# Two batches of local attention, a gated feed-forward stage and an ELU feed-forward stage: the second batch's attention issued among the first batch's feed-forward work

## The reference

```python
k_sum = k.reshape(B, H, 24, 32, D).max(axis=3)      # one key per block of 32
v_sum = v.reshape(B, H, 24, 32, D).mean(axis=3)
scores_l = scale * q @ k.T, kept where |i - j| < 16, else -1e9
scores_s = scale * q @ k_sum.T + log(32)
a = softmax(concat(scores_l, scores_s))             # over 768 + 24 keys
x = a @ concat(v, v_sum)                            # -> 1536 tokens x 512
h = x @ w_in                                        # 512 -> 1024
solu = h * softmax(h)
y = layernorm(solu) * g_ln @ w_out                  # 1024 -> 512
g = elu(y @ w2_in)                                  # 512 -> 2048
out = g @ w2_out                                    # 2048 -> 512
```

## Time and profile before

| | us |
|---|---|
| median of three runs | 532.42 |
| the three runs | 534.9, 532.42, 530.37 |
| profiled execution, its own time | 533.14 |
| its span in the trace | 531.4 |
| PE busy in the span | 495.5 |
| DVE, ACT, POOL busy | 234.9, 212.6, 100.5 |

### The profile page before, as it was taken

The page is one execution under the profiler, slowest core; times in us unless marked ns, Lnnn a source line. Parts: engine busy times, 40 slices in busy tenths (PEclk is TensorE's granted clock), DMA queues, the critical chain, the costliest instruction groups (busy, mean ns, idle before and its releaser), DMA issues.

```text
span 531.4 us, 8550 instructions
## 1 busy us (share of the span) xinstructions
PE 495.5 (93%) x3312; PEld 415.4 (78%) x3312; DVE 234.9 (44%) x625; ACT 212.6 (40%) x433; POOL 100.5 (19%) x92
## 2 busy tenths in 40 slices
PE   3769869896999999999999999999999999999997
PEld 2556757675879899899988888888888888888885
DVE  2536645634683454644265555433332323333331
ACT  2446746733573344544374435223222214122222
POOL 2245353510012002003444544100000000000000
PEclk9989977999999999999999999999999999999999
DMA  9999999661000000035000000002000002000002
GB/s 174 174 186 200 211 172 208 152 239 80 0 1 1 1 0 1 1 119 200 0 1 0 1 0 2 0 1 79 1 0 1 0 0 79 0 0 0 0 0 79
DMA packets 56131, 31.41 MB, mean 59 GB/s; under 512 B 50081, under 2 KB 50081, under 8 KB 55201
## 3 DMA queue, kind: packets, MB, share of 16 engines
q1 hardware_dynamic: 56096, 30.94, 25.5%
HBM read 26.61 MB, written 3.15 MB: 56 GB/s over the span
## 4 chain that ended last, share of the span: by engine, by line
PE 79%; SPq 8%; DMA 4%; DVE 3%; ACT 2%; issue 2%; POOL 1%; DVEq 0%
PE bank L825 12%; PE bank L826 12%; PE bank L827 12%; PE bank L1027 8%; PE bank L1026 8%; PE bank L1028 8%; PE bank L982 4%; PE bank L984 4%; PE bank L983 4%; DMA vw<-vmean 2%; PE bank L902 2%; SPq L275 2%; PE bank L968 2%; DMA vblocks<-in_v 2%; SPq L288 2%
## 5 line engine op out<-in xcount | busy, mean ns | idle before, releaser
L586 ACT ACTIVATE ex<-bank 128x512 f32<-128x512 f32 x48 | 28.7, 598 | 127.9 <-PE bank L827 127.9
L827 PE MATMUL bank<-yt_lo,w2in_hi 128*128 (+1 forms) x192 | 74.7, 389 | 0.0
L826 PE MATMUL bank<-yt_hi,w2in_lo 128*128 (+1 forms) x192 | 74.7, 389 | 0.0
L1026 PE MATMUL bank<-w2out_hi,g_hi 128*128 128x512 f32 x192 | 74.7, 389 | 0.0
L1027 PE MATMUL bank<-w2out_lo,g_hi 128*128 128x512 f32 x192 | 74.7, 389 | 0.0
L825 PE MATMUL bank<-yt_hi,w2in_hi 128*128 (+1 forms) x192 | 74.7, 389 | 0.0
L1028 PE MATMUL bank<-w2out_hi,g_lo 128*128 128x512 f32 x192 | 74.7, 389 | 0.0
L803 DVE TENSOR_SCALAR ex<-ex 128x512 f32<-128x512 f32 x48 | 21.6, 450 | 116.4 <-ACT ex L586 116.4
L808 DVE TENSOR_TENSOR g_lo<-gf,g_hi 128x512 fp32r<-128x512 f32 x48 | 46.5, 969 | 35.9 <-ACT g_hi L594 35.9
L594 ACT ACTIVATE g_hi<-gf 128x512 fp32r<-128x512 f32 x48 | 30.3, 632 | 49.0 <-DVE gf L805 49.0
L469 ACT ACTIVATE se<-se,nm 128x120 f32<-128x120 f32 x96 | 32.5, 387 | 38.6 <-DVE nm L654 38.6
(11 more groups left out here) (102 smaller groups left out, 820.3 us busy)
## 6 DMA issues: line engine op xcount, KB each, us to landing
w2in_raw<-in_w_in SPq DMA_DIRECT2D x1, 4096.0 KB, 12.4
w2out_raw<-in_w_out SPq DMA_DIRECT2D x4, 1024.0 KB, 9.4
kraw<-in_k SPq DMA_DIRECT2D x16, 192.0 KB, 4.1
qraw<-in_q SPq DMA_DIRECT2D x16, 192.0 KB, 4.1
vblocks<-in_v SPq DMA_DIRECT2D x4, 768.0 KB, 7.9
vw<-in_v SPq DMA_DIRECT2D x16, 192.0 KB, 5.6
out<-osb SPq DMA_DIRECT2D x12, 256.0 KB, 2.1
win_raw<-in_w_in SPq DMA_DIRECT2D x4, 512.0 KB, 6.1
```

The costliest lines, as they stand in the source:

```text
L826: pe.matmul(acc, al, bh, start=False, stop=False)
L827: last = pe.matmul(acc, ah, bl, start=False, stop=(i == n - 1))
L1026: pe.matmul(dst, g_hi[:, j % GS, cols], w2out_hi[:, j, :], start=(j == 0), stop=False)
```

## The change

The steps of attention stay, but from step 25 on they carry other work. Tables say at which step a row product (`ROWS_AT`), a pair of turns (`TURNS_AT`), a slice of y (`Y_AT`) and a group's factors (`STATS_AT`) are issued: rows 0 to 7, turns 0 to 15 and six of the eight y slices of groups 0 and 1 go into steps 25 to 50. Rows 8 to 11, the last two slices and turns 16 to 31 come after, in the manner of before. `y_slice(g, o)` is new: it makes one output slice of a group over all eight `f` in one go, 24 matmuls of 384 columns, in place of `y_product` after every turn.

For this, memory is laid out anew. From unit 25 on all scores go to one set of banks; the transposes of k, q and x are halved or kept at 384 columns, called pieces, and share a bank `psR`, which from step 36 on is the bank of `psP`; `psH`, `psT` and `psY` of groups 0 and 1 are one buffer each; `eh` has one buffer in place of two, `se` three in place of four, raw k and q together three in place of four, v two (a third for one pair). POOL normalises all rows; the order of the weights' DMAs is another.

```diff
+        def psS(u, h):
+            return bank(4 + h) if u < U0 and u % 2 == 1 else bank(h)
+        psO, psP = bank(2), bank(3)
+        def psR(u):
+            return bank(6 + u % 2) if u < U0 + T else bank(7) if u < U0 + 2 * T else bank(3)
+        def psH(m):
+            return banks[0] if m in (7, 9) else banks[2]
+        def psT(c):
+            return bank(2) if c >= 2 * KF and c % 2 == 1 else bank(6)
+        def psY(g, o):
+            return bank(7) if g < 2 else bank((7, 3, 0, 1)[o])
...
+        ROWS_AT = {25: 0, 27: 1, 29: 2, 31: 3, 33: 4, 37: 5, 49: 6, 50: 7}
+        TURNS_AT = {33: (0, 1), 34: (2, 3), 35: (4, 5), 36: (6, 7), 42: (8, 9), 43: (10, 11), 44: (12, 13), 45: (14, 15)}
+        Y_AT = {38: (0, 0), 39: (0, 1), 40: (0, 2), 41: (0, 3), 46: (1, 0), 48: (1, 1)}
+        SOLU_AT = {u + 1: m for u, m in ROWS_AT.items()}
+        STATS_AT = {31: 0, 39: 1}
+        AFTER = [(8, [(1, 2)], []), (9, [(1, 3)], [16]), (10, [], [17, 18]), (11, [], list(range(19, TURNS)))]
```

SP's loads of weights, in its loop over the pairs:

```diff
+                if n in (1, 2):
+                    load_win(2 * n - 2)
+                    load_win(2 * n - 1)
+                if n in (2, 3):
+                    load_vblocks(n)
+                if n in (3, 4):
+                    load_wout(2 * n - 6)
+                    load_wout(2 * n - 5)
```

ACT's step `u`; where it asks for a piece, `copy_k`, `copy_q` or `copy_x` of 384 columns follows:

```diff
+                if turns:
+                    high_turned(turns[0])
                 if u < UNITS:
                     exps(u)
                 if u >= T_LAG and u - T_LAG < UNITS and not pt_on_dve(u - T_LAG):
                     copy_pt(u - T_LAG)
+                if u in SOLU_AT:
+                    h_square(SOLU_AT[u])
+                if u in STATS_AT:
+                    deviation(STATS_AT[u])
+                if piece(u):
...
+                if turns:
+                    high_turned(turns[1])
+                if u in ROWS_AT:
+                    h_exp(ROWS_AT[u])
+                if u in Y_AT:
+                    high_y(*Y_AT[u])
```

DVE's step `u` has, each where the tables ask for it: `low_turned` of the first turn, `score(u)`, `row_solu`, `copy_pt(u-2)`, `normalise`, `variance`, `block_maxima`, `low_x`, `layernorm_factors`, `low_turned` of the second turn, `row_max`, `low_y`. PE's waits and its step (where it asks for a piece, `prep_k`, `prep_q` or `turn_x` into `psR(u)` follows):

```diff
             def scores(u):
...
                 if u >= 2:
-                    pe.wait_ge(scored, u - 1)
+                    pe.wait_ge(scored, u - 1 if u <= U0 else u)
...
             def turn_probs(u):
+                s, v = u % RING, u + T_LAG - 1
                 pe.wait_ge(expd, u + 1)
                 if u >= 1:
                     pe.wait_ge(*pt_copied(u - 1))
+                if v >= U0 + 2 * T and piece(v):
+                    pe.wait_ge(*piece_done(v))
...
             def turn(c):
...
+                if 1 <= c <= 2 * KF:
+                    pe.wait_ge(lnt_lo_ready, c)
...
+            def y_slice(g, o):
+                if g == 0 and o == 0:
+                    pe.wait_ge(wout_split, KF // 2)
+                else:
+                    pe.wait_ge(y_lo_ready, KD * g + o)
+                pe.wait_ge(lnt_lo_ready, KF * (g + 1))
...
+            for u in range(U_STEPS):
+                turns = TURNS_AT.get(u, ())
+                if turns:
+                    turn(turns[0])
+                if u < UNITS:
+                    scores(u)
+                if u >= T_LAG and u - T_LAG < UNITS:
+                    turn_probs(u - T_LAG)
+                if u >= PV_LAG and u - PV_LAG < UNITS:
+                    attend(u - PV_LAG)
+                if piece(u):
+                    kind, n, f = piece(u)
+                    if piece_before(u) is not None:
+                        pe.wait_ge(*piece_done(piece_before(u)))
+                    if u >= U0 + 2 * T:
+                        pe.wait_ge(*pt_copied(min(u - T_LAG, UNITS - 1)))
...
+                if u in ROWS_AT:
+                    rows_product(ROWS_AT[u], 0)
+                if turns:
+                    turn(turns[1])
+                if u in ROWS_AT:
+                    rows_product(ROWS_AT[u], 1)
+                if u in Y_AT:
+                    y_slice(*Y_AT[u])
```

More of the change, by code:

```diff
@@ L142, in bank @@
             return banks[i // 2][:, (i % 2) * 512:(i % 2) * 512 + 512]
[L144 to L156, removed]
+        def psS(u, h):
[9 more added lines that the diff above has]
+            return bank(7) if g < 2 else bank((7, 3, 0, 1)[o])
+        psG = [bank(4), bank(5)]
+        psA = [bank(6), bank(2), bank(7), bank(3)]
         def sem(name):
@@ L319, in _ @@
             load_k(1)
+            load_vblocks(1)
             load_q(1)
@@ L571, in _ @@
                     high_turned(c)
+                    if ends_group(c):
+                        for o in range(KD):
+                            high_y(c // KF - 1, o)
                     if TURNS - 6 <= c < TURNS - 1:
@@ L774, in _, with low_y @@
-            for m, turns in ROWS_AND_TURNS:
-                t = list(turns)
-                if m != TG + 1:
-                    row_max(m)
-                if m == TG:
-                    variance(0)
-                if t and not ends_group(t[0]):
+            def low_y(g, o):
+                tiles = slice(TG * g, TG * (g + 1))
+                dve.wait_ge(y_hi_ready, KD * g + o + 1)
+                dve.tensor_tensor(yt_lo[:, tiles, o, :], psY(g, o)[:, 0:GT].rearrange("p (t c) -> p t c", t=TG),
+                                  yt_hi[:, tiles, o, :].bitcast(F32), ALU.subtract).then_inc(y_lo_ready, 1)
@@ new lines, in _ @@
+            block_maxima(0)
+            dve.wait_ge(consts_ready, 2)
+            dve.wait_ge(vblocks_loaded[0], 16)
+            step(dve.tensor_reduce(vmean[:, 0, :], vblocks[:, 0, :].rearrange("p (w d) -> p d w", d=D), AX.X, ALU.add))
+            dve.tensor_scalar(vmean[:, 0, :], vmean[:, 0, :], 1.0 / BLOCK, None, ALU.mult).then_inc(first_vmean_ready, 1)
+            for u in range(U_STEPS):
+                n, t = u // T, u % T
+                turns = TURNS_AT.get(u, ())
+                if turns:
+                    low_turned(turns[0])
+                if u < UNITS:
+                    score(u)
+                if u in SOLU_AT:
+                    row_solu(SOLU_AT[u])
+                if u >= T_LAG and u - T_LAG < UNITS and pt_on_dve(u - T_LAG):
+                    copy_pt(u - T_LAG)
+                if u >= PV_LAG and (u - PV_LAG) % TG == TG - 1 and u - PV_LAG < UNITS:
+                    normalise((u - PV_LAG) // TG)
+                if u in STATS_AT:
+                    variance(STATS_AT[u])
+                if t == 3 and n + 1 < PAIRS:
+                    block_maxima(n + 1)
+                if u <= U0 and piece(u - 1) and piece(u - 1)[0] == "x":
+                    low_x(piece(u - 1)[1], psR(u - 1))
+                if u >= U0 and piece(u) and piece(u)[0] == "x":
+                    low_x(piece(u)[1], psR(u))
+                if u in STATS_AT:
+                    layernorm_factors(STATS_AT[u])
+                if turns:
+                    low_turned(turns[1])
+                if u in ROWS_AT:
+                    row_max(ROWS_AT[u])
+                if u in Y_AT:
+                    low_y(*Y_AT[u])
```

538 lines of the change are left out of this document (256 added, 282 removed).

## The result

The changed kernel took 589.36 us (median of four runs, 587.94 to 592.82) against 531.45: a ratio of 1.1105, 95% interval [1.1058, 1.1153]. The forecast was 556, range 538 to 570: the direction was right, the size too small by 33 us.

The account below looks back on a forecast made before the run. Attention was taken as bound by a PE, DVE, ACT, PE chain in list order, not PE's busy share. Batch 0 61, steps 24 to 51 159, after 70, second stage 264.7, outside 1.7: 556 us, range 538 to 570.

Parts of the forecast that it names:

- Reading past the busy share: Whole kernel: PE's 93% busy misleads; attention runs at a PE, DVE, ACT, PE chain, priced by the engines' lists.
- the first rival: Interleaved steps: waits vanish and PE stays the bound, 114 us there, 511 us in all; chance 0.13.
- Steps 24 to 51: Interleaved attention steps up to row 8: 159 us, of which 114 is PE's own work and the rest waiting.
- the clock: New waits in the interleaved steps: a lower clock would cost 0 to 5 us, taken as 0.
- The rest and the second stage: After step 51: 70 us to the second feed-forward stage, then 264.7 us for that stage, as before.
- 61 us, same units, smaller copies: Batch 0's attention, steps 0 to 23: 61 us, before 63.5; bounds 6 less and 4 more.
- a unit 24 later than 66: Sign at the start of unit 24's scores: after 66 us, the DMA order is the cause, not the chain.
- The last rival: Steps 34, 38 and 42: the clock falls as well, some 8 us low each, 570 us in all; chance 0.15.

Follow-up runs that it names:

- copies first: Changed kernel with v block 1's DMA order restored and batch 0's transposes in sixes, ACT and DVE serving the next step's copies before row work: 561.65 us against 569.32.
- filled kernels: Ten spare transposes in each of steps 35, 36, 42 to 45, on the changed kernel with DMA order and sixes restored: 570.85 us; with copies first too: 553.3.

## Why the prediction was right and wrong

*Reading past the busy share* was right. PE's 93% hid nothing, and the gain that a free PE would have left, the first rival's 511, did not come: ACT and DVE at 37 and 40% busy held PE up by the order of their lists. Putting copies first, with no work removed, gave back 9.6 us in these steps; that is shown, in one run.

*Steps 24 to 51* had the right mechanism and a term too small: to row 4's end 59.2 us for 55.0, to row 5's 29.5 for 27.2, slices 33.2 for 31.1, steps 42 to 46 28.4 for 25.3, steps 47 to 51 20.5 for 20.6. The sum missed by 11.8 us, 7%. The term is the clock, for which I had taken 0 from bounds 0 to 5, because ACT and DVE pace those steps. The table above prices most of it: steps 24 and 25, which began at batch 0's low level, took 3.0 us more than at the full one, and filling the waits took 5.6 us off steps 35 to 46. That is an estimate of 8.6 of the 11.8; the other 3 are not accounted for.

*The rest and the second stage* came within 0.3 us each.

*The step that failed is batch 0*, "61 us, same units, smaller copies": 80.9. I had looked for a change in its waits and transfers, gave it bounds of 6 less and 4 more, and put the clock there at nothing: I dealt with it only for steps with a long wait. What I passed over is that the change cuts the six transposes in a row of a prep into three and three. In the trace before, the low stretch that began at 34.6 had such a six in it and was over at 41.5; I read that as the clock coming back by itself:

```profile
37.54 1.54 PE L853 MATMUL bank<-ident,qraw 128*128 128x128 f32 x6
```

The two opposite edits show the step: six in a row in the changed kernel took 11.7 us off batch 0, three and three in the kernel before put 31 us on, and spare transposes that made six again took 23 of them off.

I had also written that a unit 24 later than 66 would mean the DMA order. That holds for the smaller part: restoring it alone took 7.2 us off batch 0, the sixes alone 11.7, both 15.7 of the 19.9. What is left, 65.2, is 4.2 above the forecast, just past the bound of 4.

*The last rival* had the clock in it, at three waits in the interleaved steps, and 570. In those steps it was partly right: 17.1 us of steps 34 to 37 and 20.5 of 42 to 46 were at the low level, though by the filled kernels they cost 4 to 6 us and not some 14. The larger loss, in batch 0, it did not name, nor its mechanism: a wait can start the low level, but there it lasted while the work had no long run of transposes.

The Trainium skill, TensorE: Matmul & The Clock Gate, section What's actually happening, says that the clock is set by how busy PE has been recently, and that being busy releases it. The traces here agree only if busy does not mean the busy share of the profile: 96% of it went with 1.2 GHz, 78% with 2.4.

## What to carry to other kernels

Before cutting a run of dense PE work into pieces, look whether the granted clock rises at that run; if small matmuls fill the rest, the pieces may leave PE at half clock for tens of us. When one stage's work is issued among another's, price it by each engine's list: what stands ahead of the copy that PE waits for, not how busy the engine is. Interleaving two stages that both run on PE lost time here: 10 units and 5 rows took 56 us interleaved, where alone they take 5 x 5.44 + 10 x 1.7 = 44.

## What the runs showed of the hardware

- At half clock a step of attention took 2.75 us instead of 1.6 to 1.8, and the level held for 65 us with no PE wait over 0.6 us behind its start.
- 84 added transposes of 128 columns made a kernel 23 us faster (564.61 to 541.71).
- The PEclk figures of a trace begin with the first change that it recorded: in the kernel with the DMA order restored they read 1.00 up to 86.9 us, though `attend` took 0.70 us until 66. The duration of a known matmul is the check: one of 65 columns is shown as 315 ns at the low level and 222 ns at the high one (medians in that trace up to 60 us and from 67 to 78).
